# Whole-row loads of q, a mirrored k^T v, and new orders for the attention head of a one-core kernel

## The chip, the cores and the metric

One core of one Trainium2 chip runs the whole program. The metric is the device time of one execution in microseconds (us). The engines are PE (matmul; PEld its weight loads), DVE (vector), ACT (scalar), POOL (GpSimd), and SP, which here only issues DMAs.

## The reference

An attention-like layer feeds two gated MLPs. What is computed, cut to what matters:

```python
# q, k, v: (8, 8, 576, 64) float32
kv = np.einsum('bhsd,bhse->bhde', k, v)
out = np.einsum('bhsd,bhde->bhse', q, kv)
rms = np.sqrt(np.mean(out * out, axis=-1, keepdims=True) + 1e-06)
out = (out / rms * g_norm).astype(np.float32)
x = out.transpose(0, 2, 1, 3).reshape(4608, 512)
# _moe: d_model 512, d_ff 1536
x = ((1 / (1 + np.exp(-(x @ w_gate)))) * (x @ w_val)) @ w_out
# _moe2
g = x @ w2_gate
out = (g * (1 / (1 + np.exp(-g))) * (x @ w2_val)) @ w2_out
```

## The kernel before

**The MLPs.** They are Strassen-Winograd products (seven products, numbered 1 to 7, in place of eight) of operands that are split into a high and a low part of type fp32r, so each product takes three matmuls (high by high, high by low, low by high) of 128x384. The tokens go in six blocks of 768. A stage `qq` is one block in one of three passes of one MLP; it has three windows `w`: gate, value and down projection. `g` counts windows over the whole program. A window has 14 slots (a product and a side, the order in `ORDER`) of two steps of three matmuls, 28 steps or 84 matmuls in all. All of them are issued at line L845. ACT copies products out of PSUM (`copy`, L1042), DVE adds them (`total`, L1399), multiplies gate and value (`hidden`, L1417), and ACT and DVE make the high and low parts of weights (`split_w`: L898, L1255), of x (`split_x`: L911, L1260) and of the hidden values (`hop_split`).

**The attention.** It goes in 32 units of two heads. Unit `u` does on PE:
- `unit_kv_qT(u)`: k^T v of both heads (L687, twelve matmuls) and the transposes of q (L692, six);
- `unit_o(u)`: q times k^T v (L702, twelve matmuls with 64 rows each);
- `unit_xT(u)`: transposes of the normalised result (L714, six).

Each float32 matmul or transpose outside the products may be two passes in the trace. Around these, ACT copies k^T v and the transposed q to SBUF (L921, L922), squares the result (`unit_sq`, L940), and copies x transposed (`unit_xT`); DVE sums the squares and scales (`unit_norm` L1272, `unit_scale` L1289); POOL takes the power -1/2 (`rsqrt`, L1607), and makes the weights' differences (`differences`). `keep_warm` at L671 is a matmul on constants whose result nobody reads, called a filler below; `FILLERS` says how many stand ahead of each unit's k^T v, and six more stand before three `unit_o`.

**What sets the order.** Nothing is scheduled by a tool. Each engine has its own list of calls, written out by hand, for the head (all before the first product), for window g = 0 and for window g = 1; from g = 2 on it is a rule. On PE the tables `KVQ_FIRST`, `O_FIRST` and `XT_FIRST` give, for g = 0 and g = 1, the step after which a unit's part is put in. The engines meet at semaphores. SP issues the loads in the order of the calls and waits in that order too. k and v have three buffer sets, q has two, so the load of q for unit u waits until the transposes of unit u - 2 are done (`qT_made`). All units up to 7 must be through `unit_xT` before DVE can form the sums of x (`x_s1_s3`), which products 5, 6, 7, 4 and 3 of the first block need. `load_unit(u)` issues k, v (L415) and then q in two DMAs (L421).

Of the kernel before, what the change touches and what calls it, by code (L numbers as in the profile page):

```python
# [59 lines left out]
def strassen_mlps(nc, q, k, v, g_norm, w_gate, w_val, w_out, w2_gate, w2_val, w2_out, out):  # L60
# [25 lines left out]
    q_src = q.rearrange("b h (p c) d -> (b h) p c d", c=CH)  # L86
# [9 lines left out]
    with ExitStack() as ctx:  # L96
# [289 lines left out]
        FILLERS = {0: 4, 1: 4, 2: 4, 3: 2, 4: 1, 5: 1, 7: 1}  # L386
# [16 lines left out]
        def _(sp):  # L403
            def load_unit(u):
# [264 lines left out]
        def _(pe):  # L669
# [3 lines left out]
            def unit_kv_qT(u):  # L673
# [1022 lines left out]
```

## Time and profile before

| what | us |
|---|---|
| median of 3 runs (lowest, highest) | 1740.92 (1739.97, 1741.15) |
| the profiled execution, its own time | 1741.19 |
| its span, first to last instruction | 1738.8 |
| PE busy in the span | 1717.6 |
| DVE / ACT / POOL busy | 1204.9 / 890.0 / 376.1 |

The profiled execution's time is 2.4 us above its span, and 0.27 us above the median of the runs. The share of busy time is a mean over the whole; the head of the program (here the first 47 us) and the first two windows are a few per cent of it and look different.

### The profile page before, as it was taken

The page shows a single profiled execution, that of the slowest core. Times are in us where ns is not written, and L with a number is a line of the kernel's source. Part 1 is how long each engine was busy: PE and PEld are TensorE (multiplying, and loading weights), DVE is VectorE, ACT ScalarE, POOL GpSimd, SP SyncE. Part 2 cuts the span into 40 slices and gives each one's busy share as a digit, 9 for nine tenths or more (in the row PEclk, how much of TensorE's full clock was granted, in tenths as well). Part 3 has the DMA queues.
Part 4 walks back from the last instruction along what each step waited for, and adds up shares of the span by engine and source line. Part 5 has one row for each costly group of instructions (what it writes and reads, how often), then busy time and mean ns, then how long its engine had stood idle before and what let it go on. Part 6 is the DMA issues. An engine that isn't in the chain of part 4 may idle for free.

```text
span 1738.8 us, 30846 instructions
## 1 busy us (share of the span) xinstructions
PE 1717.6 (99%) x11190; PEld 1686.7 (97%) x11190; DVE 1204.9 (69%) x1938; ACT 890.0 (51%) x1709; POOL 376.1 (22%) x326
## 2 busy tenths in 40 slices
PE   8899999999999999999999999999999999999998
PEld 7899999999999999999999999999999999999998
DVE  4876677787666678666679877787666668655556
ACT  5666666555444445444456555555444445444444
POOL 5822222013111125111136000013111124111111
PEclk9999999999999999999999999999999999999999
DMA  9887887586555567555556555576555566555553
GB/s 232 252 264 209 277 254 211 211 298 229 200 200 200 200 222 250 197 198 199 195 188 216 195 198 199 199 250 241 201 198 197 200 220 238 167 180 186 184 187 97
DMA packets 200150, 366.91 MB, mean 211 GB/s; under 512 B 49984, under 2 KB 160064, under 8 KB 200000
## 3 DMA queue, kind: packets, MB, share of 16 engines
q1 hardware_dynamic: 199776, 364.56, 62.8%
q8 instruction: 89, 1.46, 0.3%
q14 instruction: 61, 0.50, 0.1%
q10 hardware_dynamic: 224, 0.39, 0.1%
HBM read 234.36 MB, written 130.55 MB: 210 GB/s over the span
## 4 chain that ended last, share of the span: by engine, by line
PE 93%; DVE 2%; DMA 2%; issue 1%; SPq 0%; POOL 0%; ACT 0%; DVEq 0%; ACTq 0%; POOLq 0%
PE ps L845 87%; PE ps L702 2%; PE ps L687 1%; DMA wops<-in_v_dram 1%; PE ps L692 1%; PE ps L714 1%; PE ps L768 1%; DVE arena L1399 1%; DVE wa L1255 0%; DMA arena<-in_q_dram 0%; DVE arena L1417 0%; DVE xo L1260 0%; PE ps L671 0%; SPq L415 0%; DMA g<-in_g_norm_dram 0%
## 5 line engine op out<-in xcount | busy, mean ns | idle before, releaser
L845 PE MATMUL ps<-xo,wa 128*128 128x384 f32 x6048 | 1076.4, 336 | 4.4 <-DVE arena L1399 1.9
L845 PEld LDWEIGHTS ps<-xo,wa 128*128 128x128 f32 x6048 | 1045.8, 188 | 8.2 <-issue 3.4
L1042 ACT ACTIVATE arena<-ps 128x384 f32<-128x384 f32 x648 | 316.9, 491 | 574.0 <-PE ps L845 572.5
L1399 DVE TENSOR_TENSOR arena<-ps,arena 128x384 f32<-128x384 f32 x648 | 352.3, 553 | 359.0 <-PE ps L845 282.6
L845 PE MATMUL ps<-hop,wb 128*128 128x384 f32 x3024 | 537.9, 335 | 1.2 <-DVE arena L1417 0.9
L845 PEld LDWEIGHTS ps<-hop,wb 128*128 128x128 f32 x3024 | 523.0, 188 | 4.9 <-issue 2.5
L1670 POOL TENSOR_TENSOR arena<-arena 128x384 f32<-128x384 f32 x144 | 146.8, 1045 | 734.9 <-DVE arena L1399 734.9
L1349 DVE TENSOR_TENSOR hop<-arena,hop 128x384 fp32r<-128x384 f32 (+1 forms) x396 | 275.3, 718 | 33.9 <-ACT hop L1024 28.0
L1024 ACT ACTIVATE hop<-arena 128x384 fp32r<-128x384 f32 (+1 forms) x396 | 233.5, 609 | 61.1 <-DVE arena L1417 33.4
L1056 ACT ACTIVATE arena<-arena 128x384 f32<-128x384 f32 x216 | 112.5, 521 | 66.6 <-DVE arena L1399 66.6
L1417 DVE TENSOR_TENSOR arena<-arena 128x384 f32<-128x384 f32 x216 | 129.2, 600 | 20.3 <-DVE arena L1399 1.4
L1607 POOL TENSOR_TENSOR rrms<-msq,mhalf 96x12 f32<-96x12 f32 x32 | 91.0, 2847 | 189.5 <-DVE msq L1275 189.5
L1612 POOL TENSOR_TENSOR wops<-wops 128x256 f32<-128x256 f32 x36 | 32.4, 901 | 423.9 <-DMA wops<-in_moe_w_gate_dram 272.4
L1260 DVE TENSOR_TENSOR xo<-xraw,xo 128x768 fp32r<-128x768 f32 x60 | 59.7, 1005 | 6.6 <-ACT xo L911 6.4
L1255 DVE TENSOR_TENSOR wa<-wops,wa 128x768 fp32r<-128x768 f32 (+1 forms) x48 | 55.4, 1180 | 11.2 <-ACT wa L898 10.9
L911 ACT ACTIVATE xo<-xraw 128x768 fp32r<-128x768 f32 x60 | 49.3, 841 | 13.4 <-DVE xraw L1307 12.2
L1417 DVE TENSOR_TENSOR arena<-arena,ps 128x384 f32<-128x384 f32 x72 | 39.6, 550 | 23.1 <-PE ps L845 22.9
L1366 DVE TENSOR_TENSOR arena<-arena 128x384 f32<-128x384 f32 x72 | 41.6, 578 | 7.4
L898 ACT ACTIVATE wa<-wops 128x768 fp32r<-128x768 f32 (+1 forms) x48 | 43.8, 946 | 1.8 <-POOL wops L1617 1.8
L1357 DVE TENSOR_TENSOR arena<-arena 128x384 f32<-128x384 f32 x72 | 41.5, 576 | 2.5
L1361 DVE TENSOR_TENSOR arena<-arena 128x384 f32<-128x384 f32 x72 | 41.9, 582 | 0.0
L1614 POOL TENSOR_TENSOR wops<-wops 128x256 f32<-128x256 f32 x36 | 41.2, 1145 | 2.8
(75 smaller groups left out, 779.4 us busy)
## 6 DMA issues: line engine op xcount, KB each, us to landing
xo<-x_operands SPq DMA_DIRECT2D x168, 768.0 KB, 6.2
x_operands<-xo SPq DMA_DIRECT2D x84, 768.0 KB, 5.2
x<-arena SPq DMA_DIRECT2D x120, 384.0 KB, 2.9
arena<-x SPq DMA_DIRECT2D x96, 384.0 KB, 4.5
xraw<-x SPq DMA_DIRECT2D x22, 768.0 KB, 6.3
wops<-in_moe_w_gate_dram SPq DMA_DIRECT2D x24, 256.0 KB, 5.1
wops<-in_moe_w_val_dram SPq DMA_DIRECT2D x24, 256.0 KB, 4.5
wops<-in_moe_w_out_dram SPq DMA_DIRECT2D x48, 128.0 KB, 2.3
```

The source lines that it names most:

```text
L845: mm = pe.matmul(dst, lhsT, rhs, start=(pr in (1, 5, 2) and c == 0 and i == 0), stop=(c == 1 and i == 2), skip_group_check=(pr in (6, 7, 4 ...
L911: nc.scalar.activation(xo[:, pr - 1, HI], x_source(pr), ACT.Copy).then_inc(x_hi, 1)
L1024: nc.scalar.activation(hop_place(pr, c, HI), hop_source(pr, c), ACT.Copy).then_inc(hop_hi, 1)
L1042: nc.scalar.activation(dst, X(side), ACT.Copy).then_inc(copied, 1)
L1056: nc.scalar.activation(dst, src, (ACT.Sigmoid, ACT.Silu)[l]).then_inc(sig_done, 1)
L1255: nc.vector.tensor_tensor(dst[:, at, LO, :], wops[:, unit % 2, at], dst[:, at, HI, :].bitcast(F32), ALU.subtract).then_inc(w_lo, 1)
L1260: nc.vector.tensor_tensor(xo[:, pr - 1, LO], x_source(pr), xo[:, pr - 1, HI].bitcast(F32), ALU.subtract).then_inc(x_lo, 1)
L1349: nc.vector.tensor_tensor(hop_place(pr, c, LO), hop_source(pr, c), hop_place(pr, c, HI).bitcast(F32), ALU.subtract).then_inc(hop_lo, 1)
L1399: nc.vector.tensor_tensor(dst, acc, buf, ALU.add).then_inc(summed, 1)
L1417: nc.vector.tensor_tensor(dst, gate, val, ALU.mult).then_inc(h_done, 1)
L1607: nc.gpsimd.tensor_tensor(rrms[:, u % 2], msq[:, u % 2], mhalf[:], ALU.pow).then_inc(rrms_ready, 1)
L1670: nc.gpsimd.tensor_tensor(dst, buf, res[:, t, half, side], ALU.add).then_inc(part_added, 1)
```

## The change

- **q.** `q_src` has the layout of `k_src`: one DMA for both heads of a unit, rows of 384 elements (1536 bytes) where there were rows of 64 elements (256 bytes). In SBUF q is then ordered by head, chunk, element, and a transpose takes two chunks of one head rather than one chunk of two heads.
- **k^T v.** Since each half of the partitions now holds chunks of either head, each half needs k^T v of both heads. ACT writes it three times: as before, and two copies of 64x64 with the halves swapped. `unit_o` has the same count of matmuls. `unit_sq`, `unit_scale` and `unit_xT` read and write the new layout.
- **Loads.** `load_unit` falls into `load_kv` and `load_q`; in the head, q of a unit is issued behind k and v of the next one in most places, the first weights come later, and the small load of g is no longer ahead of ACT's first copies.
- **Fillers.** 15 stand ahead of nine units' k^T v and 3 between the first `unit_kv_qT` and `unit_o` (18 in all) where there were 17 and 6 (23).
- **Orders.** Head, g = 0 and g = 1 have new lists on all engines; `unit_o(8)` and `unit_xT(6)` move behind the first product's step.

The core of the diff:

```diff
-    q_src = q.rearrange("b h (p c) d -> (b h) p c d", c=CH)
+    q_src = q.rearrange("b h (p c) d -> p (b h) (c d)", c=CH)
-        FILLERS = {0: 4, 1: 4, 2: 4, 3: 2, 4: 1, 5: 1, 7: 1}
+        FILLERS = {0: 4, 1: 1, 2: 2, 3: 2, 4: 1, 5: 1, 6: 1, 7: 2, 8: 1}
-        KVQ_FIRST = ({5: 9, 15: 10}, {11: 11})
+        KVQ_FIRST = ({5: 9, 17: 10}, {13: 11})
...
-                for h in range(2):
-                    sp.dma_start(q_in(u)[:, :, h * D:(h + 1) * D], q_src[2 * u + h]).then_inc(q_loaded[u % 2], 16)
+                sp.dma_start(q_in(u), q_src[:, 2 * u:2 * u + 2, :]).then_inc(q_loaded[u % 2], 16)
...
             load_unit(0)
-            load_unit(1)
+            load_kv(1)
+            load_kv(2)
+            load_q(1)
+            load_w(0)
+            load_q(2)
             for d in (0, D):
                 sp.dma_start(g2[d:d + D, :], g_norm.rearrange("(d a) -> d a", a=1)).then_inc(g_loaded, 16)
...
-                for c in range(CH):
-                    mm = pe.transpose(ps[:, b + c // HALF, c % HALF * SP_:(c % HALF + 1) * SP_], q_in(u)[:, c, :],
-                                      ident[0:SP_, 0:SP_])
+                for h in range(2):
+                    for j in range(HALF):
+                        mm = pe.transpose(ps[:, b + h, j * SP_:(j + 1) * SP_], q_in(u)[:, h, j * P:(j + 1) * P],
+                                          ident[0:SP_, 0:SP_])
...
-                nc.scalar.activation(kv_sb(u), ps[:, b + 1, HALF * SP_:HALF * SP_ + D], ACT.Copy).then_inc(kv_copied, 1)
+                kv = ps[:, b + 1, HALF * SP_:HALF * SP_ + D]
+                nc.scalar.activation(kv_sb(u)[:, 0:D], kv, ACT.Copy)
+                nc.scalar.activation(kv_sb(u)[0:D, D:2 * D], kv[D:2 * D], ACT.Copy)
+                nc.scalar.activation(kv_sb(u)[D:2 * D, D:2 * D], kv[0:D], ACT.Copy).then_inc(kv_copied, 1)
...
-            act.wait_ge(g_loaded, 32)
             unit_kv_qT(0)
+            unit_sq(0)
             unit_kv_qT(1)
-            unit_sq(0)
-            unit_sq(1)
             split_w(0, RAW)
             unit_kv_qT(2)
+            unit_sq(1)
+            act.wait_ge(g_loaded, 32)
             unit_xT(0)
```

On PE, the start of the head stands before as follows (L671 filler, L687 k^T v, L692 q transposed, L702 `unit_o`, L714 `unit_xT`):

```order
1 L671 MATMUL ps<-xs,ident 128x256 x4
2 L687 MATMUL ps<-arena 64x64 x12
3 L692 MATMUL ps<-ident,arena 128x96 x6
4 L671 MATMUL ps<-xs,ident 128x256 x4
5 L687 MATMUL ps<-arena 64x64 x12
6 L692 MATMUL ps<-ident,arena 128x96 x6
7 L702 MATMUL ps<-att_o,arena 96x64 x24
8 L671 MATMUL ps<-xs,ident 128x256 x4
9 L687 MATMUL ps<-arena 64x64 x12
```

and in the changed kernel (L685 filler, L701 k^T v, L708 q transposed, L721 `unit_o`, L734 `unit_xT`):

```order
1 L685 MATMUL ps<-xs,ident 128x256 x4
2 L701 MATMUL ps<-arena 64x64 x12
3 L708 MATMUL ps<-ident,arena 128x96 x6
4 L685 MATMUL ps<-xs,ident 128x256 x3
5 L721 MATMUL ps<-att_o,arena 96x64 x12
6 L685 MATMUL ps<-xs,ident 128x256
7 L701 MATMUL ps<-arena 64x64 x12
8 L708 MATMUL ps<-ident,arena 128x96 x6
9 L685 MATMUL ps<-xs,ident 128x256 x2
10 L701 MATMUL ps<-arena 64x64 x12
11 L708 MATMUL ps<-ident,arena 128x96 x6
12 L721 MATMUL ps<-att_o,arena 96x64 x12
```

`unit_o(0)` moved ahead of unit 1, and ahead of unit 2's k^T v stand ten fillers in four places where there were twelve in three.

SP's queue at its start before (in_k, in_v: L415; q: L421; the small load of g; the first weights):

```order
1 L415 DMA arena<-in_k_dram 96x2x384
2 L415 DMA arena<-in_v_dram 96x2x384
3 L421 DMA arena<-in_q_dram 96x6x64 x2
4 L415 DMA arena<-in_k_dram 96x2x384
5 L415 DMA arena<-in_v_dram 96x2x384
6 L421 DMA arena<-in_q_dram 96x6x64 x2
7 L511 DMA g<-in_g_norm_dram 64x1 x2
8 L445 DMA wops<-in_moe_w_gate_dram 128x4x128 x2
9 L415 DMA arena<-in_k_dram 96x2x384
```

and in the changed kernel:

```order
1 L416 DMA arena<-in_k_dram 96x2x384
2 L416 DMA arena<-in_v_dram 96x2x384
3 L423 DMA arena<-in_q_dram 96x2x384
4 L416 DMA arena<-in_k_dram 96x2x384
5 L416 DMA arena<-in_v_dram 96x2x384
6 L416 DMA arena<-in_k_dram 96x2x384
7 L416 DMA arena<-in_v_dram 96x2x384
8 L423 DMA arena<-in_q_dram 96x2x384
9 L451 DMA wops<-in_moe_w_gate_dram 128x4x128 x2
10 L423 DMA arena<-in_q_dram 96x2x384
11 L521 DMA g<-in_g_norm_dram 64x1 x2
```

q of unit 1 moved behind k and v of unit 2, q of unit 2 behind the first weights.

DVE in the second half of the changed kernel's g = 0 and the start of g = 1, where the changed kernel has the split of the down projection's weights (into `wb`, now L1268, four in a row) ahead of the first `total` of g = 1 (now L1412), and the split of x in between (L1273):

```order
68 L1302 TENSOR_TENSOR arena<-arena,rrms 96x768
69 L1268 TENSOR_TENSOR wb<-wops,wb 128x3x256
70 L1268 TENSOR_TENSOR wb<-wops,wb 128x4x256
71 L1268 TENSOR_TENSOR wb<-wops,wb 128x3x256
72 L1268 TENSOR_TENSOR wb<-wops,wb 128x4x256
73 L1273 TENSOR_TENSOR xo<-xraw,xo 128x768
```

where DVE before had the first of the four in g = 0 and the first `total` of g = 1 (L1399) ahead of the split of x:

```order
67 L1361 TENSOR_TENSOR arena<-arena 128x384
68 L1255 TENSOR_TENSOR wb<-wops,wb 128x4x256
69 L1255 TENSOR_TENSOR wb<-wops,wb 128x3x256
70 L1255 TENSOR_TENSOR wb<-wops,wb 128x4x256
71 L1399 TENSOR_TENSOR arena<-ps,arena 128x384
```

All four weight splits now stand in g = 1.

## Rows read from the trace of the kernel before

**Rows 1.** The page: busy time by engine, share of the span, instructions

```profile
PE 1717.6 (99%) x11190; PEld 1686.7 (97%) x11190; DVE 1204.9 (69%) x1938; ACT 890.0 (51%) x1709; POOL 376.1 (22%) x326
```

**Rows 2.** Windows: stretch, its length, busy PE, PEld, DVE, ACT, POOL, clock, DMA share, GB/s

```profile
0.00:47.10 47.10, 41.58 (x575) 34.11 (x575) 21.61 (x31) 24.96 (x47) 25.38 (x22) 1.00 1.12 236
...
60.00:75.00 15.00, 13.95 (x122) 13.23 (x121) 14.47 (x19) 10.04 (x19) 11.64 (x8) 1.00 0.57 181
...
95.10:1700.00 1604.90, 1599.32 (x10048) 1579.88 (x10048) 1114.92 (x1809) 814.72 (x1570) 308.37 (x278) 1.00 0.62 212
```

**Rows 3.** Waits of PE in 0 to 95.1: four and the last of 11

```profile
PE ps L714 <- DVE arena L1289: 2.3, 2, 1.2
PE ps L692 <- DMA arena<-in_q_dram: 1.6, 3, 0.8
PE ps L671 <- POOL ident L1599: 1.5, 1, 1.5
PE ps L702 <- ACT arena L922: 1.2, 1, 1.2
...
PE ps L845 <- DVE arena L1417: 0.2, 1, 0.2
```

**Rows 4.** Groups of instructions on PE in 0 to 100, shapes apart: busy, mean ns

```profile
L702 PE MATMUL ps<-att_o,arena 64*96 64x64 f32 x288 | 14.6, 248 | 1.9 <-ACT arena L922 1.2 <-ACT att_o L921 0.7
L671 PE MATMUL ps<-xs,ident 128*128 128x256 f32 x46 | 13.9, 436 | 1.8 <-POOL ident L1599 1.5 <-ACT arena L954 0.2
...
L687 PE MATMUL ps<-arena 96*64 96x64 f32 x264 | 10.1, 226 | 1.1 <-ACT arena L963 0.8 <-DMA arena<-in_v_dram 0.3
```

**Rows 5.** Timeline of PE: start, duration of the run of instructions, idle before it

```profile
1.52 3.57 PE L671 MATMUL ps<-xs,ident 128*128 128x256 f32 x8 [1.52 <-POOL ident L1599]
...
7.05 1.92 PE L671 MATMUL ps<-xs,ident 128*128 128x256 f32 x8
...
11.90 2.25 PE L702 MATMUL ps<-att_o,arena 64*96 64x64 f32 x48 [0.68 <-ACT att_o L921]
...
25.14 0.71 PE L692 MATMUL ps<-ident,arena 96*128 96x96 f32 x6 [0.75 <-DMA arena<-in_q_dram]
...
44.36 1.13 PE L671 MATMUL ps<-xs,ident 128*128 128x256 f32 x4 [0.24 <-ACT arena L954]
...
49.62 0.71 PE L714 MATMUL ps<-ident,arena 96*128 96x96 f32 x6 [1.24 <-DVE arena L1289]
...
73.41 2.32 PE L845 MATMUL ps<-xo,wa 128*128 128x384 f32 x12 [0.22 <-DVE arena L1417]
...
92.14 1.33 PE L845 MATMUL ps<-xo,wa 128*128 128x384 f32 x6 [0.63 <-DVE arena L1399]
```

**Rows 6.** Timeline of ACT: its first copies

```profile
10.99 0.22 ACT L921 ACTIVATE att_o<-ps 128x64 f32<-128x64 f32 x1 [8.76 <-DMA g<-in_g_norm_dram]
11.11 0.64 ACT L922 ACTIVATE arena<-ps 128x576 f32<-128x576 f32 x1
```

**Rows 7.** DMA, 4.5 to 6.0: nearly only q's rows

```profile
DMA packets 847, 0.33 MB, mean 219 GB/s; under 512 B 754, under 2 KB 847, under 8 KB 847
```

**Rows 8.** DMA, 2.5 to 4.0: nearly only rows of k and v

```profile
DMA packets 352, 0.46 MB, mean 308 GB/s; under 512 B 57, under 2 KB 352, under 8 KB 352
```

**Rows 9.** DMA issues in 0 to 100: count, KB each, median us to landing

```profile
arena<-in_k_dram SPq DMA_DIRECT2D x11, 288.0 KB, 5.5
...
arena<-in_q_dram SPq DMA_DIRECT2D x22, 144.0 KB, 5.5
```

**Rows 10.** Groups on the other engines in 0 to 100

```profile
L1607 POOL TENSOR_TENSOR rrms<-msq,mhalf 96x12 f32<-96x12 f32 x12 | 35.6, 2976 | 25.8 <-DVE msq L1275 25.8
...
L1272 DVE TENSOR_REDUCE ssum<-arena 96x12 f32<-96x768 f32 x8 | 7.6, 947 | 18.9 <-ACT arena L940 18.9
...
L940 ACT ACTIVATE arena<-ps 96x768 f32<-96x768 f32 x8 | 6.5, 807 | 4.9 <-PE ps L714 3.3 <-PE ps L702 1.5
...
L1255 DVE TENSOR_TENSOR wb<-wops,wb 128x1024 fp32r<-128x1024 f32 x2 | 2.4, 1211 | 0.0
```

More of the change, by code:

```diff
@@ L403, in _, with load_kv @@
         def _(sp):
-            def load_unit(u):
+            def load_kv(u):
                 if u > EARLY:
@@ L723, in _ @@
             unit_kv_qT(0)
+            for _ in range(3):
+                keep_warm(att_bank(1))
+            unit_o(0)
             unit_kv_qT(1)
-            unit_o(0)
+            unit_kv_qT(2)
             unit_o(1)
-            unit_kv_qT(2)
             unit_xT(0)
@@ L733, in _ @@
             unit_o(3)
+            unit_o(4)
             unit_xT(2)
-            unit_o(4)
             unit_kv_qT(5)
-            pe.wait_ge(xT_ready, 3)
-            for _ in range(2):
-                keep_warm(att_bank(6))
+            unit_kv_qT(6)
+            unit_xT(3)
             unit_o(5)
-            unit_xT(3)
-            unit_kv_qT(6)
-            unit_xT(4)
             unit_kv_qT(7)
             unit_o(6)
-            pe.wait_ge(xT_ready, 5)
-            for _ in range(2):
-                keep_warm(att_bank(8))
+            unit_xT(4)
             unit_o(7)
@@ L751, in _ @@
             unit_kv_qT(8)
-            pe.wait_ge(xT_ready, 6)
-            for _ in range(2):
-                keep_warm(att_bank(5))
-            unit_o(8)
-            unit_xT(6)
             def turn(qq, i):
@@ L978, in _ @@
             unit_kv_qT(3)
+            split_w(1, RAW)
             unit_kv_qT(4)
@@ L981, in _ @@
             unit_sq(3)
-            split_w(1, RAW)
             unit_sq(4)
@@ L1316, in _ @@
             unit_norm(0)
-            unit_norm(1)
             unit_scale(0)
             split_w(0, RAW)
+            unit_norm(1)
             unit_norm(2)
+            split_w(0, SUMMED)
             unit_scale(1)
-            split_w(0, SUMMED)
+            split_w(1, RAW)
             unit_scale(2)
@@ L1326, in _ @@
             unit_scale(3)
-            split_w(1, RAW)
+            split_w(1, SUMMED)
+            unit_norm(5)
             unit_scale(4)
-            unit_norm(5)
             split_x(0, 1)
-            split_w(1, SUMMED)
             unit_scale(5)
@@ L1335, in _ @@
             unit_scale(6)
+            split_w(2, RAW)
+            unit_scale(7)
             split_x(0, 2)
-            unit_scale(7)
-            split_w(2, RAW)
             unit_norm(8)
@@ L1617, in differences @@
                 nc.gpsimd.tensor_tensor(st[:, 2], st[:, 6], st[:, 1], ALU.subtract).then_inc(t_made, 1)
+            def differences(unit):
+                differences_1_3(unit)
+                differences_2_4(unit)
             rsqrt(0)
```

194 lines of the change are left out of this document (105 added, 89 removed).

## The prediction

> **What bounds the kernel now.** I read the page's busy times first: PE is busy 1717.6 us of the span of 1738.8 [rows 1], at a granted clock of 1.00 in every stretch, which of the two levels (1.2 and 2.4 GHz) is 2.4 [rows 2]. So the time is PE's work plus what PE loses, and the question is where it loses. The windows answer: from 95.1 to 1700 PE idles 5.6 us in 1605, while from 0 to 47.1, where the first product starts, it is busy 41.6 of 47.1 [rows 2]. 95.1 us is also where both orders have done the same work (all of g = 0 and g = 1, units 0 to 11 up to `unit_o`, `unit_xT` up to 10, three steps of g = 2), and from there on the lists are the same. So I cost the change up to that point only.
>
> The loss there has two parts. The waits of PE sum to 10.4 us over the 11 entries of the chain of waits by line; 1.5 us of it, before the first filler, stays [rows 3]. The remaining **8.9 us** could go. The fillers are 46 passes, 13.9 us [rows 4]. The first eight took 3.57 us, with nothing on PE before them, later eight 1.92 us [rows 5]: a warm filler of two passes costs about 0.5 us from start to start. With no waits and 5 fillers fewer, the gain is 8.9 + 2.5 = 11.4 us. That is one end.
>
> **The change, part by part.**
>
> *Work on PE.* k^T v, q's transposes, `unit_o`, `unit_xT` keep their counts: 288 passes of `unit_o` and 264 of k^T v stand in the rows for 12 and 11 units, 24 a unit, about 1.2 and 0.9 us [rows 4], and the two lots of transposes take 0.71 each [rows 5]. `unit_o` still alternates between the halves of the partitions. Cost: nothing either way.
>
> *Fillers.* 23 become 18: 5 x 0.5 = **-2.5 us**, if nothing else is waited for in their place.
>
> *q in whole rows.* Nearly pure traffic of q's 256-byte rows went at 219 GB/s, of k's and v's rows at 308 GB/s [rows 7, 8]. q of a unit is 288 KB (two DMAs of 144 KB [rows 9]), 0.295 MB: 1.35 us before, 0.96 after, 0.4 us saved per unit. In the head the DMA share is full (1.12 over 47.1 us) [rows 2], so for nine units about 3.5 us of transfer time go. Only three waits for q, 1.6 us, show on PE [rows 3]; the rest is time by which later loads come earlier. The Trainium skill, "DMA: Bandwidth & Descriptors", section "Why small descriptors are slow (HBM only)", prices the overhead of a 256-byte descriptor at 27%; by that the saving would be near 0.3 us per unit, 2.6 us for nine. The trace's two rates differ by 41%, so the trace makes it dearer than the page. Against it speaks the median from issue to landing, 5.5 us for 144 KB of q and for 288 KB of k alike [rows 9]: what is waited for is a backlog.
>
> *Two more copies on ACT per unit.* Not in the trace in this shape. The nearest row is L921: 0.22 us busy, but the next instruction starts 0.12 us after it [rows 6]. Between 2 x 0.12 and 2 x 0.22; I take 0.24 us per unit, since they stand back to back. From g = 2 on ACT is busy half of the time (814.7 of 1604.9) [rows 2] and the copies are asked for steps ahead of `unit_o`: nothing. Were that cover gone, 20 late units x 0.24 = 4.8 us.
>
> *g no longer waited for.* ACT idled 8.76 us for it and copied at 10.99 [rows 6], though PE had finished with unit 0 when it began unit 1's fillers at 7.05 [rows 5]. Now `unit_o(0)` can follow at about 8.2 (transposes to 6.8, three fillers) instead of 11.90 [rows 5], and its chain (square 0.8, sum 0.95, power 3.0 in the mean [rows 10], a scaling about as long as the sum) starts 3.7 us earlier.
>
> *The new orders, walked through.* I followed the lists with the durations above. Landings I took as 2 us + 1.04 x the transfer time queued ahead + 1.5 us, which gives 24.0 for q of unit 4 before, where the trace has 25.14 [rows 5].
> - q of unit 1 now stands behind k, v of unit 2: lands at 11.7, PE ready at 10.8, **0.9** lost. q of unit 2 stands behind the first weights: 15.3 against 14.3, **1.0**.
> - ACT has `split_w(1, RAW)` ahead of `unit_kv_qT(4)` and so waits for weights until 24: `unit_o(4)` **0.5** late.
> - Units 6 and 7: PE comes earlier than before and meets the DMA backlog: **1.2** and **0.8**.
> - The transposes of unit 8 end at 43.5, against 44.1 before (the filler behind them, at 44.36, had waited 0.24 [rows 5]): so far the gain is only 0.6 us; the head is bound by loads.
> - Then PE is freed: before, it lost two fillers, a wait of 1.2 ahead of `unit_xT(7)` at 49.62 [rows 5] and 0.2 more. Now `unit_o(8)` and `unit_xT(6)` stand behind a product's step, and `unit_xT(7)` starts at 46.7: **2.9 us** earlier.
> - From there DVE sets the pace (busy 14.5 of 15 us from 60 to 75 [rows 2]). Product 6 waits for its split behind `unit_scale(8)`, itself behind POOL's power, which stands behind four differences: **0.8**.
> - `unit_o(10)` now stands in g = 0; the wait of 0.8 for `unit_norm(10)` ahead of `unit_xT(9)` goes, since the sum stands in g = 0 now. Step 2 of g = 1, at 73.41 before [rows 5], comes at 69.
> - In g = 1 DVE has four weight splits (1.2 each [rows 10]) and two splits of x ahead of `total(22, 0)`, for which the 22nd step's product waits: I get **1.2**, and **0.3** for `unit_xT(10)`. Step 26, at 92.14 before [rows 5], comes at about 87.5.
>
> Sum of the new waits: 0.9 + 1.0 + 0.5 + 1.2 + 0.8 + 0.1 + 0.8 + 1.2 + 0.3 = **6.8 us**. Gain: 2.5 + 8.9 - 6.8 = **4.6 us**. The profiled execution took 1741.19, 0.27 above the median of the runs; 1741.19 - 4.6 = 1736.6, against the median 1740.92 - 4.6 = **1736.3 us**.
>
> **The rivals.** What a measurement can tell from no change is about 0.2%, 3.5 us.
>
> 1. *As worked out*, a gain of 3.5 to 6.5 us: 1734.4 to 1737.4. Chance 0.56.
> 2. *The orders fit better than my walk.* The 4.4 us of waits for loads and for ACT up to unit 8 are estimates on a backlog; if loads land 1 us earlier each they halve, and if DVE's waits in g = 1 are hidden too, 2.5 are left: gain 8.9, 1732.0. For it: the backlog shrinks by 3.5 us over the head. Against it: DVE is full after 50 us whatever PE does. Chance 0.13.
> 3. *The gain is eaten by DVE or by loads.* Every stall in front moves only to where DVE is full: fillers go, but the new waits come to 8.5 or more. If landings come no earlier than before (5.5 us from issue for either size), the head ends at 44.1 and the two later estimates double. Gain 0 to 3.5 us, 1739 in the middle. Chance 0.22.
> 4. *Slower: the TensorE clock falls in the head.* Fewer fillers stand between 7 and 30 us, ahead of waits of 0.9 and 1.0. In the trace of before the clock stayed full over waits of up to 1.2 us [rows 3]. If it falls to 1.2 GHz, work on PE takes up to 3.57 / 1.92 = 1.9 times as long [rows 5]: from 12 to 30 us about 13 us of attention work would take up to 12 us more, 1740.9 + 12 - 4.6 = 1748. It decides from about 5 us of such work. Chance 0.04.
> 5. *Slower: ACT.* If the copies do stand in `unit_o`'s way from g = 2 on, 20 units x 0.24 = 4.8 us eat the gain, and at 0.44 each (8.8) the kernel is 4.2 us slower, 1745. Against it: PE waited for ACT only 1.2 us at one `unit_o` before 95 (an entry of [rows 3]). Chance 0.05.
>
> **How the numbers follow.** The predicted time is that of case 1, 1736.3. Cases 1 to 3 cover 1732.0 to 1740.9. The range 1732.0 to 1739.6 leaves out the upper part of case 3 and cases 4 and 5, less than 0.2 together. Faster by over 0.2% (below 1737.4): cases 1 and 2, 0.69. Within 0.2%: case 3 and some of 5, 0.24. Slower: 0.07.
>
> **What would show it.** PE's waits up to the common point sum to about 7 us plus the first 1.5, fillers come to 36 passes. `unit_o(0)` starts near 8.2. q lands sooner, and the rate between 4.5 and 6 is near 300 GB/s. The first product starts at 43 to 44, step 26 of g = 1 at 87 to 88; from 95 on PE idles as before, about 5 to 6 us. Wrong would be: waits of PE for DVE's `total` and the splits that make up more than 4 us after 50 us (case 3), passes of L685 or L701 near twice their warm time after 6 us, or a granted clock below full (case 4), entries of PE on ACT's L934 to L936 after 95 us (case 5).

## The result and the profile after

| | before | changed |
|---|---|---|
| median of 7 runs each | 1740.92 us | 1746.72 us |
| lowest and highest | 1739.97, 1741.15 | 1741.28, 1752.45 |
| profiled execution | 1741.19, span 1738.8 | 1743.13, span 1741.3 |
| start of unit 12's k^T v in it | 95.1 | 97.1 |

The ratio is 1.0036, with an interval of 1.0026 to 1.0046: slower, by 5.8 us between the medians, where 4.6 us less were forecast. The spread is news too: 11 us, where before it was 1.2 in seven executions. Each execution also comes with its mean granted clock, and the seven line up by it:

```
1741.28 0.998   1743.13 0.998   1744.16 0.995   1746.72 0.993
1746.93 0.992   1750.72 0.990   1752.45 0.989
```

A line through these and the 12 of the repeat below, 19 executions of the same kernel, has 1.03 us more for each 0.001 less of mean clock, ends at 1740.1 us for full clock, and the two go together closely (correlation -0.97). The 137 executions of the kernel before that were measured beside the experiments give 1739.9 at full clock; their mean clock was 0.999, and they spread from 1737.85 to 1750.57, so the kernel before meets the fall too, but seldom. So there are two things to explain: why the clock falls, and why even at full clock nothing was gained.

The page of the changed kernel says as little as that of before [rows 1]:

```profile
PE 1718.1 (99%) x11180; PEld 1686.4 (97%) x11180; DVE 1203.9 (69%) x1938; ACT 906.0 (52%) x1773; POOL 364.6 (21%) x326
```

Its windows show the granted clock (the column ahead of the DMA share):

```profile
6.00:12.00 6.00, 5.65 (x80) 4.49 (x76) 0.68 (x1) 2.12 (x5) 0.00 (x0) 1.00 1.11 235
12.00:20.00 8.00, 6.68 (x76) 5.46 (x78) 2.67 (x4) 3.90 (x10) 5.86 (x5) 0.79 1.12 257
20.00:30.00 10.00, 8.91 (x151) 7.71 (x148) 6.46 (x9) 7.48 (x17) 8.35 (x6) 1.00 1.12 255
...
90.00:1700.00 1610.00, 1603.25 (x10071) 1583.34 (x10071) 1119.03 (x1819) 828.53 (x1617) 308.62 (x279) 1.00 0.62 213
```

From 12 to 20 us it is 0.79 in the mean, so a part of it was at 1.2 GHz; in the other windows up to 1700 us it is full (in the last 41 us 0.96), and past 90 PE idles 6.8 of 1610 us, as before [rows 2]. The timeline of PE shows what stood around the fall:

```profile
11.01 0.92 PE L701 MATMUL ps<-arena 96*64 96x64 f32 x24
13.32 0.82 PE L708 MATMUL ps<-ident,arena 96*128 96x96 f32 x6 [1.40 <-DMA arena<-in_q_dram]
13.93 1.97 PE L685 MATMUL ps<-xs,ident 128*128 128x256 f32 x4
15.83 1.53 PE L701 MATMUL ps<-arena 96*64 96x64 f32 x24
17.29 0.71 PE L708 MATMUL ps<-ident,arena 96*128 96x96 f32 x6
```

PE waits 1.40 us for q of unit 1. The four filler passes behind it take 1.97 us and unit 2's k^T v 1.53, which was 0.92 a unit earlier. Then six transposes take 0.71 again. A mean of 0.79 over 8 us is 8 x 0.21 x 2 = 3.4 us at half clock.

The waits of PE up to 95 us, which answer to [rows 3]:

```profile
PE ps L708 <- DMA arena<-in_q_dram: 5.1, 3, 1.9
PE ps L685 <- POOL ident L1612: 1.5, 1, 1.5
PE ps L856 <- DVE arena L1412: 1.5, 1, 1.5
PE ps L721 <- ACT arena L936: 1.4, 2, 1.1
PE ps L856 <- ACT arena L1053: 0.8, 1, 0.8
PE ps L685 <- ACT arena L967: 0.7, 1, 0.7
PE ps L856 <- DVE arena L1430: 0.4, 1, 0.4
...
```

With one of 0.3 left out they sum to 11.7 us, 10.2 without the first filler's 1.5, where 6.8 were forecast and 8.9 stood before. The largest is q, three times, up to 1.9. The groups of PE up to the common point give the rest of the account, beside [rows 4]:

```profile
L856 PE MATMUL ps<-xo,wa 128*128 128x384 f32 x168 | 33.7, 346 | 2.9 <-DVE arena L1412 1.5 <-ACT arena L1053 0.8 <-DVE arena L1430 0.4
...
L685 PE MATMUL ps<-xs,ident 128*128 128x256 f32 x36 | 12.8, 486 | 2.2 <-POOL ident L1612 1.5 <-ACT arena L967 0.7
L701 PE MATMUL ps<-arena 96*64 96x64 f32 x264 | 11.4, 243 | 0.0
```

The fillers are 36 passes, as forecast, but 12.8 us against 13.9: 1.1 us less, not 2.5, since some ran at half clock. The same 264 passes of k^T v take 11.4 us instead of 10.1, half of it in unit 2 at half clock and half in unit 0, whose k^T v took 1.55 us at 5.35 where it was 0.92 at 5.13 before. The 168 passes of the products take 33.7 us, and 32.3 before. In all, PE was busy 85.1 us and idle 12.0 up to the common point at 97.1; before it was 84.5 and 10.6 up to 95.1. With a mean clock of 0.998 this is one of the milder executions.

### The profile page after: what moved, and what is told of

Read it like the earlier page. It is cut to its first block, busy times and chain, and to the rows that moved or that the text cites. A ratio compares the mean times of both kernels' runs of the same rounds, so it can differ in the third digit from the quotient of the medians.

```text
span 1741.3 us, 30857 instructions
## 1 busy us (share of the span) xinstructions
PE 1718.1 (99%) x11180; PEld 1686.4 (97%) x11180; DVE 1203.9 (69%) x1938; ACT 906.0 (52%) x1773; POOL 364.6 (21%) x326
## 4 chain that ended last, share of the span: by engine, by line
PE 92%; DVE 3%; DMA 2%; issue 1%; SPq 1%; ACT 0%; POOL 0%; DVEq 0%; ACTq 0%; POOLq 0%
PE ps L856 86%; PE ps L721 2%; PE ps L701 1%; DMA arena<-in_q_dram 1%; PE ps L708 1%; PE ps L779 1%; PE ps L734 1%; DVE arena L1412 1%; DMA wops<-in_v_dram 0%; DVE wb L1268 0%; DVE wa L1268 0%; DVE xo L1273 0%; DVE hop L1362 0%; DMA wops<-in_moe_w_out_dram 0%; DVE arena L1430 0%
## 5 line engine op out<-in xcount | busy, mean ns | idle before, releaser
L856 PEld LDWEIGHTS ps<-xo,wa 128*128 128x128 f32 x6048 | 1045.6, 188 | 10.7 <-DVE arena L1412 3.8
L1412 DVE TENSOR_TENSOR arena<-ps,arena 128x384 f32<-128x384 f32 x648 | 351.9, 553 | 358.2 <-PE ps L856 281.1
L1035 ACT ACTIVATE hop<-arena 128x384 fp32r<-128x384 f32 (+1 forms) x396 | 233.4, 608 | 62.4 <-DVE arena L1430 33.7
L1620 POOL TENSOR_TENSOR rrms<-msq,mhalf 96x12 f32<-96x12 f32 x32 | 85.5, 2675 | 200.5 <-DVE msq L1288 200.4
L1625 POOL TENSOR_TENSOR wops<-wops 128x256 f32<-128x256 f32 x36 | 29.5, 819 | 426.5 <-DMA wops<-in_moe_w_gate_dram 273.6
L1268 DVE TENSOR_TENSOR wa<-wops,wa 128x768 fp32r<-128x768 f32 (+1 forms) x48 | 56.1, 1194 | 14.0 <-ACT wa L909 13.6
L1273 DVE TENSOR_TENSOR xo<-xraw,xo 128x768 fp32r<-128x768 f32 x60 | 59.1, 997 | 7.4 <-ACT xo L922 7.4
L1285 DVE TENSOR_REDUCE ssum<-ps 96x12 f32<-96x768 f32 x24 | 22.9, 952 | 25.1 <-ACT ps L953 25.1
```

Source lines behind the costliest of these rows:

```text
L856: mm = pe.matmul(dst, lhsT, rhs, start=(pr in (1, 5, 2) and c == 0 and i == 0), stop=(c == 1 and i == 2), skip_group_check=(pr in (6, 7, 4 ...
L1035: nc.scalar.activation(hop_place(pr, c, HI), hop_source(pr, c), ACT.Copy).then_inc(hop_hi, 1)
L1268: nc.vector.tensor_tensor(dst[:, at, LO, :], wops[:, unit % 2, at], dst[:, at, HI, :].bitcast(F32), ALU.subtract).then_inc(w_lo, 1)
L1273: nc.vector.tensor_tensor(xo[:, pr - 1, LO], x_source(pr), xo[:, pr - 1, HI].bitcast(F32), ALU.subtract).then_inc(x_lo, 1)
L1412: nc.vector.tensor_tensor(dst, acc, buf, ALU.add).then_inc(summed, 1)
L1620: nc.gpsimd.tensor_tensor(rrms[:, u % 2], msq[:, u % 2], mhalf[:], ALU.pow).then_inc(rrms_ready, 1)
```

## The experiments

Each result gives the median, in brackets the number of executions and sometimes the lowest and highest, then the ratio to the kernel before on the same chip with its 95% interval, then the clock, which is the mean over the executions of the kernel. The "common point" is the start of unit 12's k^T v, up to which all versions have done the same work.

**1. The changed kernel again, and the fillers' numbers.** `r_after` is the changed kernel unchanged. 

> The changed kernel again, unaltered, on the chip of the other three. Clock theory (PE's clock falls to 1.2 GHz in the head, at another place in each execution): the times spread over several us again, 1741 to 1752, and each execution's time goes up as its mean granted clock goes down from 0.998. Load theory (q's order on SP costs, the clock is a side matter): the same median near 1745, with a spread below 3 us.

`e_more_fill` gives units 1 and 2 of the changed kernel the fillers of before, `e_few_fill` the kernel before the changed kernel's fewer.

```diff
 # e_more_fill, on the changed kernel
-        FILLERS = {0: 4, 1: 1, 2: 2, 3: 2, 4: 1, 5: 1, 6: 1, 7: 2, 8: 1}
+        FILLERS = {0: 4, 1: 4, 2: 4, 3: 2, 4: 1, 5: 1, 6: 1, 7: 2, 8: 1}
 # e_few_fill, on the kernel before
-        FILLERS = {0: 4, 1: 4, 2: 4, 3: 2, 4: 1, 5: 1, 7: 1}
+        FILLERS = {0: 4, 1: 1, 2: 2, 3: 2, 4: 1, 5: 1, 7: 1}
```

> The changed kernel with four fillers ahead of units 1 and 2 again (five more, 2.5 us of PE work at full clock). Clock theory: the mean clock stays at 0.999 or above, the spread shrinks to below 2 us, and the median falls to 1741 to 1743 in spite of the added work. Load theory: fillers only fill waits for q, 1744 to 1747, no better than the changed kernel. If fillers are plain cost: 2.5 us above the changed kernel.

> The kernel before with one filler ahead of unit 1 and two ahead of unit 2, as in the changed kernel (five fewer), and nothing else changed. Clock theory: the granted clock falls below 1 in some executions and the times spread upwards, 1740 to 1750. If five fillers are only work on the path: 1738.4, 2.5 us faster. If they only fill waits: 1741.

Measured: `r_after` 1744.58 us (12 runs, 1739.97 to 1752.73), 1.0024 [1.0013, 1.0035], clock 0.995. `e_more_fill` 1744.82 (11), 1.0021 [1.0011, 1.0030], 0.9955. `e_few_fill` 1742.22 (11), 1.0019 [1.0003, 1.0036], 0.996, with two executions at 1753 where the clock was 0.988 and 0.989. So the five fillers alone, in the old orders, already bring some of the excess. The traced execution of `r_after` took 1752.73 us and shows the dear case. Windows:

```profile
20.00:30.00 10.00, 8.11 (x93) 6.72 (x93) 5.50 (x6) 5.44 (x13) 7.88 (x6) 0.70 1.12 254
30.00:40.00 10.00, 10.00 (x98) 8.35 (x97) 3.64 (x6) 4.65 (x9) 6.45 (x5) 0.50 0.84 208
40.00:50.00 10.00, 10.00 (x90) 8.49 (x90) 4.54 (x6) 4.94 (x12) 3.68 (x3) 0.50 0.35 90
50.00:60.00 10.00, 10.00 (x83) 8.68 (x81) 4.67 (x7) 5.94 (x12) 5.23 (x3) 0.50 0.47 129
60.00:75.00 15.00, 15.00 (x133) 13.90 (x132) 10.64 (x15) 11.44 (x21) 5.72 (x5) 0.83 0.55 192
```

and timeline of PE at the fall and at the first product:

```profile
20.49 0.92 PE L701 MATMUL ps<-arena 96*64 96x64 f32 x24
23.30 0.71 PE L708 MATMUL ps<-ident,arena 96*128 96x96 f32 x6 [1.89 <-DMA arena<-in_q_dram]
...
24.65 1.55 PE L701 MATMUL ps<-arena 96*64 96x64 f32 x24
26.13 1.22 PE L708 MATMUL ps<-ident,arena 96*128 96x96 f32 x6
...
58.07 1.31 PE L856 MATMUL ps<-xo,wa 128*128 128x384 f32 x3
```

Here the wait of 1.40 was 0.67 and PE kept its clock; a wait of 1.89 us for q of unit 3 came instead, and behind it k^T v takes 1.55 and the transposes 1.22 for 0.71. Then the clock stays at 0.50 from 30 to 60 us, though PE is busy 10.00 of every 10 us with attention work, and it rises only at 65 us, after the first products. Worked out from the means, 6 + 30 + 5 = 41 us were spent at 1.2 GHz. The common point is at 108.0 in this trace, 12.9 us behind that of before. The DMA share falls to 0.35: once PE is the slow one, it waits for no load. Five more fillers in units 1 and 2 alone did not help the changed kernel, against the expectation: the trace of `e_more_fill` has its fall from 35 to 42 us, far behind them.

**2. Which part brings it.** `e_rows_alone` is the kernel before with q's whole rows and the k^T v on both halves; `e_orders_alone` is the changed kernel with q in 64-element rows and one copy.

```diff
 # e_rows_alone, on the kernel before (and the addressing of qT, xn and kv_sb with it)
-                for h in range(2):
-                    sp.dma_start(q_in(u)[:, :, h * D:(h + 1) * D], q_src[2 * u + h]).then_inc(q_loaded[u % 2], 16)
+                sp.dma_start(q_in(u), q_src[:, 2 * u:2 * u + 2, :]).then_inc(q_loaded[u % 2], 16)
...
-                nc.scalar.activation(kv_sb(u), ps[:, b + 1, HALF * SP_:HALF * SP_ + D], ACT.Copy).then_inc(kv_copied, 1)
+                kv = ps[:, b + 1, HALF * SP_:HALF * SP_ + D]
+                nc.scalar.activation(kv_sb(u)[:, 0:D], kv, ACT.Copy)
+                nc.scalar.activation(kv_sb(u)[0:D, D:2 * D], kv[D:2 * D], ACT.Copy)
+                nc.scalar.activation(kv_sb(u)[D:2 * D, D:2 * D], kv[0:D], ACT.Copy).then_inc(kv_copied, 1)
 # e_orders_alone: the same lines the other way, on the changed kernel
```

> The kernel before with q loaded in whole rows and the mirrored k^T v (two more copies on ACT), in the orders and with the fillers of before. If rows of 1536 bytes go at 308 GB/s in the head as I took it: the waits for q go (1.6 us), later loads come up to 3.5 us earlier, 1737 to 1740. If the DMA rate of the head stays near 245 GB/s whatever the rows: no gain from the loads, and 0.6 us more delay per unit on ACT, 1741 to 1743. Clock theory: clock 1.000, no spread.

> The changed kernel with q in rows of 64 elements again (two DMAs a unit, one copy of k^T v): only orders and fillers are new. If the new orders cause the waits for q and the fall of the clock: 1744 or more with a mean clock of 0.995. If the rows and the copies had a part in it (0.6 us more per unit on ACT): 1741 to 1743.

Measured: `e_rows_alone` 1741.29 us (11), 1.0007 [0.9998, 1.0015], clock 0.999: no gain, no loss. `e_orders_alone` 1749.95 (6), 1.0060 [1.0043, 1.0077], clock 0.993: the worst of all. So the slowness came with the orders and their fewer fillers, which this pair does not tell apart, and the rows take part of it back. The waits of PE up to 95 us have one telling entry each, here `e_rows_alone`:

```profile
PE ps L706 <- ACT arena L930: 2.8, 6, 0.7
```

and here `e_orders_alone`:

```profile
PE ps L707 <- DMA arena<-in_q_dram: 7.9, 5, 2.2
```

With the rows and the old orders PE never waits for q, but 2.8 us for ACT's copies, six times, where it was 1.9 before [rows 4]. With the new orders and the old rows it waits 7.9 us for q.

**3. q nearer, and the same fillers elsewhere.** `e_q_near` issues q right behind its own k and v for units 1, 3, 4, 6, 7 and 8. `e_fill_at_q` puts the eleven fillers of units 1 to 8 between k^T v and q's transposes, where PE waits. `e_near_and_fill` does both.

```diff
 # e_q_near, on the changed kernel
-            load_kv(1)
-            load_kv(2)
-            load_q(1)
+            load_unit(1)
+            load_kv(2)
...
-            load_kv(3)
-            load_kv(4)
-            load_q(3)
-            load_q(4)
+            load_unit(3)
+            load_unit(4)
 # e_fill_at_q
-                for _ in range(FILLERS.get(u, 0)):
+                for _ in range(FILLERS[0] if u == 0 else 0):
                     keep_warm(b)
...
+                for _ in range(FILLERS.get(u, 0) if u > 0 else 0):
+                    keep_warm(b)
                 pe.wait_ge(q_loaded[u % 2], 16 * (u // 2 + 1))
```

> The changed kernel with q of units 1, 3, 6 and 7 issued directly behind its own k and v on SP instead of behind the next unit's. If the order of the loads makes the waits for q (5.1 and 3.4 us in two traces): the waits for q fall below 1.5 us, no gap of 1.4 us or more stands ahead of a transpose, the clock stays at 0.998 or above, and the median is 1740 to 1742. If the fall of the clock has nothing to do with these waits: 1744 to 1746, mean clock near 0.995 again.

> The changed kernel with the same eleven fillers of units 1 to 8, but between a unit's k^T v and its transposes of q, where the waits for q are, instead of ahead of its k^T v. If a wait for q of 1.4 to 1.9 us with nothing on PE is what the clock falls after: each such wait is 0.5 to 1 us shorter, the clock stays nearer 1, median 1740 to 1743. If only the amount of work on PE matters: as the changed kernel, 1744.6.

> Both edits together: q behind its own k and v, and the eleven fillers ahead of q's transposes. Clock theory: clock 0.999 or above in nearly all executions, spread below 3 us, median 1739.5 to 1741, that is what the changed kernel does at full clock. Theory that the head's loads bound it: 1741 or more even at full clock.

Measured: `e_q_near` 1743.68 us (11), 1.0021 [1.0011, 1.0032], clock 0.9945. `e_fill_at_q` 1741.76 (12, up to 1752.28), 1.0010 [0.9999, 1.0021], 0.997. `e_near_and_fill` 1744.62 (7), 1.0023 [1.0010, 1.0035], 0.995. With q nearer PE waits 1.7 us for q instead of 5.1, but up to 2.1 for ACT's copies and 2.0 for DVE, and the clock falls all the same: its trace is at half from 29 us on, behind the wait for ACT, and again from 46 us on, behind the wait for DVE. So it need not be q that is waited for. Moving the fillers to the wait may help some; its interval touches 1, and `e_near_and_fill` does not bear it out.

**4. Filling the waits, and emptying them.** `e_many_fill` and `e_one_fill` add two or one filler ahead of q's transposes in units 1 to 8 of the changed kernel, 16 or 8 more, all of them added work. `e_no_fill` takes the 13 fillers behind unit 0 from the kernel before.

```diff
 # e_many_fill (e_one_fill: 1 for 2), on the changed kernel
+                for _ in range(2 if 1 <= u <= SHARED else 0):
+                    keep_warm(b)
                 pe.wait_ge(q_loaded[u % 2], 16 * (u // 2 + 1))
 # e_no_fill, on the kernel before
-        FILLERS = {0: 4, 1: 4, 2: 4, 3: 2, 4: 1, 5: 1, 7: 1}
+        FILLERS = {0: 4}
```

> The changed kernel with two more fillers between k^T v and the transposes of q in each of units 1 to 8 (sixteen more, 8 us of PE work at full clock, some of it inside the waits for q of 3.4 to 5.1 us). Clock theory: the clock stays at 0.999 or above and the spread shrinks below 3 us; the median is then set by the added work, 1740 + 8 - 3 to 5 = 1743 to 1745, with no execution above 1747. If fillers don't hold the clock: 1746 to 1753 with a mean clock of 0.995.

> The kernel before with the thirteen fillers ahead of units 1, 2, 3, 4, 5 and 7 taken out (6.5 us of PE work at full clock); the first four and the six ahead of unit_o stay. Clock theory: the clock falls in most executions, mean clock below 0.996, median 1743 to 1750 though work was taken away. If fillers were only work: down to 1737; if they only fill waits: 1741.

> The changed kernel with one more filler between k^T v and q's transposes in each of units 1 to 8 (eight more, 4 us of PE work; sixteen more gave a ratio of 1.000 at a mean clock of 0.9995). If eight are enough to hold the clock: mean clock 0.999 or above, and 1738.5 to 1740.5, a little faster than with sixteen. If not: spread to 1747 again, median above 1741.

Measured: `e_many_fill` 1741.47 us (11, 1738.27 to 1742.92), 1.0000 [0.9990, 1.0009], clock 0.9995. `e_one_fill` 1739.91 (11, 1737.28 to 1741.21), 0.9997 [0.9988, 1.0006], 0.9996. `e_no_fill` 1745.81 (5), 1.0034 [1.0021, 1.0047], 0.992. Eight fillers more take the changed kernel's excess away, and thirteen fewer give the kernel before an excess of the same size. The traces of these two and of `e_g_fill` below show no fall in the first 110 us. The groups of `e_one_fill` up to its common point, 93.7:

```profile
L685 PE MATMUL ps<-xs,ident 128*128 128x256 f32 x52 | 17.4, 448 | 2.2 <-POOL ident L1614 1.5 <-ACT arena L969 0.7
...
L701 PE MATMUL ps<-arena 96*64 96x64 f32 x264 | 10.7, 234 | 0.0
L710 PE MATMUL ps<-ident,arena 96*128 96x96 f32 x66 | 7.8, 255 | 0.6 <-DMA arena<-in_q_dram 0.4
```

52 passes and 17.4 us of fillers, 4.6 more than in the changed kernel, but the wait for q is 0.4 for 5.1, k^T v is down to 10.7, and the common point came 3.4 us earlier. (Its chip also moved loads faster, 268 GB/s from 2 to 20 us against 251; but `e_q_near`, without the added fillers, was at 1.0021 on this same chip.) And the windows of `e_no_fill`:

```profile
6.00:12.00 6.00, 3.98 (x58) 3.28 (x56) 0.00 (x0) 1.38 (x4) 0.00 (x0) 0.86 1.18 256
12.00:20.00 8.00, 7.04 (x81) 6.51 (x80) 4.02 (x6) 3.21 (x6) 4.02 (x3) 0.50 1.18 244
20.00:30.00 10.00, 10.00 (x109) 8.98 (x109) 4.10 (x6) 5.07 (x10) 9.50 (x7) 0.50 0.93 208
```

At half clock from the first gaps on, it stays there while PE is fully busy from 20 to 30. It was full again at 38 us, 14 us ahead of the first product.

**5. Single edits on the kernels with the old orders.** `e_g_late` is `e_rows_alone` with ACT's wait for g moved behind the third unit's copies; `e_g_only` does that alone to the kernel before, and `e_g_fill` adds one filler ahead of q's transposes in units 1 to 8 to it. `e_no_mirror` is `e_rows_alone` without the two new copies: half of `unit_o`'s products then use the other head's k^T v.

```diff
 # e_g_late, e_g_only
-            act.wait_ge(g_loaded, 32)
             unit_kv_qT(0)
...
             unit_kv_qT(2)
+            act.wait_ge(g_loaded, 32)
             unit_xT(0)
 # e_no_mirror, on e_rows_alone
-                nc.scalar.activation(kv_sb(u)[:, 0:D], kv, ACT.Copy)
-                nc.scalar.activation(kv_sb(u)[0:D, D:2 * D], kv[D:2 * D], ACT.Copy)
-                nc.scalar.activation(kv_sb(u)[D:2 * D, D:2 * D], kv[0:D], ACT.Copy).then_inc(kv_copied, 1)
+                nc.scalar.activation(kv_sb(u)[:, 0:D], kv, ACT.Copy).then_inc(kv_copied, 1)
```

> The kernel before with whole rows and the mirrored k^T v, and ACT's wait for g moved behind the third unit's copies. ACT starts near 7.7 instead of 10.7 us. If a chain that starts 3 us earlier is worth time: 1738 to 1739.5. If the head is bound by its loads (some 250 GB/s): as with the rows alone, 1741, since unit 2 on wait for the same bytes.

> The kernel before with one edit: ACT's wait for g behind the third unit's copies. If an earlier start of the chain is worth time at the old orders: 1738 to 1739.5 against 1740.7 to 1741.2 of before. If the head is bound by what comes later: no difference, ratio 0.999 to 1.0005.

> The same, with one more filler ahead of q's transposes in each of units 1 to 8 (eight more, 4 us of PE work). If fillers in the head are covered and guard the clock: mean clock 0.9995 or above, fewer executions above 1742 than before, median 1739 to 1740.5, the best of the case. If they are on the path at the old orders, which wait little: 1742 to 1744.

> The kernel before with whole rows of q but without the two added copies of k^T v on ACT; unit_o reads the one copy for both heads, so that half of the attention's products are formed with the other head's k^T v. The rest of the work is the same. If the two copies cost time in the head: PE's waits for ACT ahead of unit_o fall from 2.8 us to about 1.2 and the median falls by 1 to 2 us against the rows alone, 1739.5. If not: 1741.

Measured: `e_g_late` 1739.94 us (11), 0.9995 [0.9986, 1.0004], clock 0.999. `e_g_only` 1740.73 (12), 1.0018 [1.0001, 1.0035], 0.996: seven executions at 1739.5 to 1741.0, five at 1749.7 to 1752.1, nothing between. `e_g_fill` 1740.79 (12, 1739.28 to 1743.55), 0.9994 [0.9983, 1.0006], 0.9998. `e_no_mirror` 1739.40 (11), 0.9992 [0.9983, 1.0001], 0.999. So with a single edit that only lets ACT start earlier, 5 of 12 executions have the clock's fall, where of the 29 of the kernel before on this chip one was as slow (1750.57), and eight fillers take it out again. PE's wait for q in its traced execution (1752.12 us) was

```profile
PE ps L692 <- DMA arena<-in_q_dram: 1.9, 3, 1.4
```

at most 1.4, and behind it the windows read as in `r_after`:

```profile
20.00:30.00 10.00, 10.00 (x84) 7.95 (x82) 4.07 (x5) 3.28 (x6) 9.32 (x7) 0.50 0.93 217
30.00:40.00 10.00, 10.00 (x90) 8.59 (x90) 3.97 (x6) 4.68 (x10) 4.75 (x3) 0.50 0.47 112
```

Without the two copies PE waits for ACT 1.2 us in place of 2.8; in the time that is 1.9 us between medians of two chips, which the intervals do not settle.

**6. The bytes.** `e_half_q` loads q of one head only in units 3 to 8 of the changed kernel, 0.88 MB less; the other head's q is what lay there. `e_late_w` is `e_one_fill` with the third step's weights behind all of q.

```diff
 # e_half_q, on the changed kernel
-                sp.dma_start(q_in(u), q_src[:, 2 * u:2 * u + 2, :]).then_inc(q_loaded[u % 2], 16)
+                n = 1 if 3 <= u <= SHARED else 2
+                sp.dma_start(q_in(u)[:, 0:n], q_src[:, 2 * u:2 * u + n, :]).then_inc(q_loaded[u % 2], 16)
 # e_late_w, on e_one_fill
-            load_kv(6)
-            load_kv(7)
-            load_q(6)
-            load_w(2)
-            load_kv(8)
-            load_q(7)
-            load_q(8)
+            load_unit(6)
+            load_kv(7)
+            load_q(7)
+            load_kv(8)
+            load_q(8)
+            load_w(2)
             load_w(3)
```

> The changed kernel with q loaded for one of the two heads only in units 3 to 8 (0.88 MB less, 3.5 us at 250 GB/s; the other head's rows of the buffer keep an earlier unit's values, so these results are of the wrong q). If the head is bound by the bytes of its loads and the clock falls in the waits for them: the waits for q shrink from 3.4 to 5.1 us to below 2, the mean clock rises to 0.998 or above and the median falls to 1738 to 1741. If the orders themselves (the waits of SP and the engines on each other) are what binds: 1743 to 1745 and a clock near 0.995, as the changed kernel.

> The same, and on SP q of units 6, 7 and 8 directly behind their k and v, the third weights (0.52 MB, 2.1 us at 250 GB/s) behind unit 8. If bytes ahead of q are what the head waits for: the waits for q of units 6 and 7 go, the common point comes 1.5 to 3 us earlier, 1737 to 1739, the first version that beats the one before. If the chain through ACT, DVE and POOL binds there already: as with the one filler alone.

Measured: `e_half_q` 1737.40 us (11, 1736.05 to 1739.57), 0.9980 [0.9971, 0.9988], clock 0.9995. `e_late_w` 1743.11 (11), 1.0012 [1.0004, 1.0021], 0.998. `e_half_q` is the one version that gained: 3.0 us against the kernel before on its chip, and 2.7 against the changed kernel's 1740.1 at full clock, with 0.88 MB less, which take 3.5 us at 251 GB/s. Its waits for q are

```profile
PE ps L709 <- DMA arena<-in_q_dram: 4.1, 5, 1.1
```

five, none over 1.1, and the clock held. (Their sum, 4.1 us, did not shrink to below 2.) The same bytes in another order (`e_late_w`) were worse, as the timeline of PE shows:

```profile
44.88 1.01 PE L735 MATMUL ps<-ident,arena 96*128 96x96 f32 x6 [3.00 <-DVE arena L1303]
```

The wait went to the weights: POOL stood for them for 5.5 us with the power of unit 5 queued behind, so DVE's scaling came late and PE waited 3.0 us for it; the six transposes behind the wait took 1.01 us, and the clock was at half from 46 to 52 us.

## Why the prediction was wrong

**The step that failed is the rival it gave 0.04: "the TensorE clock falls in the head".** Its own mark, passes of L685 or L701 near twice their warm time after 6 us, stands in both traces. The ground for 0.04 was "in the trace of before the clock stayed full over waits of up to 1.2 us", from one execution; and the waits it forecast itself were of that size, up to 1.2. They came out at 1.40, 1.84 and 1.90 in one execution and 1.89 in the other, and falls stood behind a wait of 1.4 and one of 1.89; yet the ones of 1.84 and 1.90 in the changed kernel's own trace, at 41 and 35 us, had none behind them. So a long wait did not always bring the fall.

What the runs show is that taking fillers away brings the fall and adding them takes it off: in the kernel before the ratio is 1.0019 with 18 of its 23 fillers and 1.0034 with 10; in the changed one it is 1.0024 and 1.0036 with its 18, 0.9997 with 26 and 1.0000 with 34. Their place may count as well: with 23, of which the five more stand in units 1 and 2, it is 1.0021. And they are no full guard: `e_late_w`, with 26 and a wait of 3.0 us, is at 1.0012 with a fall in its trace. The loads weigh in too: with the old rows and the same 18 fillers it is 1.0060. The Trainium skill, "TensorE: Matmul & The Clock Gate", section "Part 1: The HAM clock gate (the "warmup" mystery)", has the chip set TensorE's clock by how busy the engine has been of late. The fillers agree with it: eight more brought the mean clock from 0.995 to 0.9996. The half clock from 30 to 60 us in `r_after`, with PE recorded as busy throughout, is not explained by it. That the rival's 1748 stands near the measured 1746.72 is in part luck: it takes off a gain of 4.6 us that was not there, and it has one fall from 12 to 30 us, where the traces have anything from 3.4 us at half clock to 41.

The price of a filler, "-2.5 us", counted only its work; 1.1 us was saved in the traced execution, and what they guarded is up to 1752.7 - 1740.1 = 12.6 us.

**Without the fall the answer was still no gain: case 3.** `e_one_fill`, with the clock full, is at 0.9997, and the line through the executions ends at 1740.1. Three terms were wrong:

- *The transfer time, 3.5 us over nine units.* The rates of [rows 7, 8] were those of the first microseconds. Over 5 to 30 us the kernel before moved

```profile
DMA packets 10874, 5.99 MB, mean 239 GB/s; under 512 B 6644, under 2 KB 10872, under 8 KB 10872
```

and the changed kernel

```profile
DMA packets 5941, 6.28 MB, mean 251 GB/s; under 512 B 507, under 2 KB 5939, under 8 KB 5939
```

5% more, which over 25 us is 1.2 us. From 2 to 20 us, where every trace has its loads queued, chips can be compared: on one chip 247 GB/s with the old rows against 246 to 259 with the new, on a second 252 against 254 to 259, on a third 256 against 259 to 275. Whole rows are worth some 3%, and the traces of one chip with the new rows differ by more than that. The sum took 219 against 308, 41%. q's short rows were at most 6644 of 256 bytes, 28% of the bytes of the stream from 5 to 30 us, so 41% on them would be some 11% on the stream, by estimate. The Trainium skill, "DMA: Bandwidth & Descriptors", section "Why small descriptors are slow (HBM only)", gives such rows an overhead of 27%, by which an estimate for the stream is 8%. Both are more than was measured.
- *The waits for q, 0.9 + 1.0 + 1.2 + 0.8 = 3.9 us.* They measured 5.1: 1.4, 1.9 and 1.8 for units 1, 6 and 7, and none for unit 2. That they follow from the term before is likely, but only argued. `e_q_near` and `e_late_w` show that another order of the same bytes moves the wait to ACT, DVE or POOL, and `e_half_q` that with fewer bytes no wait for q is over 1.1.
- *ACT's copies, 0.24 us per unit.* The bounds were 0.24 to 0.44. The timeline of ACT in the changed kernel has

```profile
7.71 0.22 ACT L933 ACTIVATE att_o<-ps 128x64 f32<-128x64 f32 x1 [5.47 <-PE ps L708]
7.95 0.22 ACT L934 ACTIVATE att_o<-ps 64x64 f32<-64x64 f32 x1
8.18 0.21 ACT L935 ACTIVATE att_o<-ps 64x64 f32<-64x64 f32 x1
8.42 0.65 ACT L936 ACTIVATE arena<-ps 128x576 f32<-128x576 f32 x1
```

0.71 us from the first copy to q's, where it was 0.12 [rows 6]: 0.59 per unit. The row used showed a small copy followed by a large one, and not small ones in a row.

A term put at nothing, PE's work, was not quite that: the products' 168 passes took 33.1 us in `e_one_fill` at full clock, and 32.3 before; the runs do not say why. Two slips in the working mattered little: the sum has a term of 0.1 that the walk does not name, and PE waited for ACT's copies ahead of `unit_o` twice before, 1.2 and 0.7 us [rows 4], not once.

**What was right, and what else was not.** g is not waited for and `unit_o(0)` started at 9.21 (8.2 forecast, 11.90 before); the copies and the first k^T v are the difference, which took 1.55 us, as long as at half clock, though the row for 2 to 6 us gives 1.00. Fillers are 36 passes. DVE's wait ahead of the 22nd step of g = 1 was 1.5 (1.2 forecast). But `unit_xT(7)` at 51.99, not 46.7, is later than before [rows 5], the first product started at 48.38 and not at 43 to 44, and step 26 of g = 1 at 94.33 and not at 87.5. Between 4.5 and 6 us the loads went at 259 GB/s, not near 300. From the common point to the end the changed kernel's span has 1644.2 us and that of before 1643.7, so nothing lies there: case 5 did not happen.

**What stays open.** Why one execution falls and another of the same kernel does not: loads that land some tenths later are likely, but only argued. Why the waits of 1.90 and 1.84 us passed without a fall was not tried. Five more fillers in units 1 and 2 did nothing for the changed kernel and eight spread over the waits did all; whether it was the number or the place, only `e_fill_at_q` tried, and its interval touches 1. No version that computes the right result beat the kernel before by what can be told: `e_one_fill`, `e_g_late` and `e_g_fill` are all within 0.1% of it.

## What to carry to other kernels

In this head, which waits for loads, eight more fillers ahead of the waits cost nothing that could be measured (0.9997 and 0.9994), since PE idled there anyway, and they guard a clock whose fall cost up to 12.6 us; before taking one away, price the fall, and look at more than one execution, since one trace at full clock doesn't show how near it was. Where loads are back to back, as here, other orders moved the wait and only fewer bytes shortened the head: count bytes. And a transfer's price is that of the mixed stream over its whole stretch, not of the purest microsecond of it.

## What the runs showed of the hardware

- Once at half, the clock stayed there for about 41 us in `r_after`, 30 of them with PE recorded as busy throughout, through transposes and fp32 matmuls of 64 columns; it was back at 65 us, after products (128 x 384) had begun at 58 us. Products are not needed for it: the fall in the changed kernel's own trace was over by 17.3 us, within attention work of the same kind, and those of `e_no_fill`, `e_fill_at_q` and `e_g_only` at 38, 38 and 43 us, 9 us or more ahead of their first products.
- The length of a wait did not settle it: waits of 2.15 and 2.17 us in `e_orders_alone` and of 1.84 and 1.90 in the changed kernel had no fall behind them, while falls stood behind waits of 1.23 (`e_fill_at_q`) and 1.03 us (`e_no_mirror`).
- Time followed the mean clock at 1.03 us per 0.001 in the changed kernel (1.17 in the kernel before).
- Three copies of 64 columns on ACT with nothing to wait for start 0.23 to 0.24 us apart, each 0.21 to 0.22 long; the large copy behind them in the kernel before started 0.12 us after the small one [rows 6].
- Rows of 256 and of 1536 bytes for q differ by some 3% in the rate of the stream, while the stream with the new rows alone ran at 246 to 275 GB/s over the traces of four chips, and at 259 to 275 on one of them.
